# Five query tiles of 128, 128, 128, 96 and 96 rows, a new order of the first loads, and unread products at TensorE's start

## What is computed

```python
q_rot, k_rot = rotate(q), rotate(k)                  # (4, 8, 576, 64)
scores = (q_rot @ k_rot.T) / sqrt(64)
attn = exp(scores - max) / (sum(exp) + 1e-9)
x = (attn @ v) as (4, 576, 512)
u = x + (x.T @ U @ V).T                              # U (576, 32), V (32, 576)
out = u + maximum(u @ w_ch1, 0) @ w_ch2              # (512, 2048), (2048, 512)
```

## Time and profile before

| | |
|---|---|
| median of 3 executions | 755.5 us (755.38 to 759.19) |
| profiled execution | 755.52 us, span 753.7 us |
| TensorE busy | 712.1 us of the span |
| VectorE, ScalarE, GpSimd busy | 407.8, 438.8, 465.4 us |
| TensorE's first product | 11.00 us |
| scores of tile 5 (first of head 1) start | 24.59 us |
| first product with v starts | 30.34 us |
| scores of tile 10 (first of head 2) start | 34.13 us |
| MLP alone from | about 600 us |

### The profile page before, as it was taken

One profiled execution on the slowest core, in us unless ns is written; L12 is line 12 of the kernel. 1 busy time (PEld: TensorE's weight loads), 2 busy tenths in 40 slices (PEclk: granted clock), 3 DMA queues, 4 the chain that ended last, 5 costly groups with the idle time before them and its releaser, 6 DMA issues.

```text
span 753.7 us, 12305 instructions
## 1 busy us (share of the span) xinstructions
PE 712.1 (94%) x4292; PEld 640.9 (85%) x4292; DVE 407.8 (54%) x676; ACT 438.8 (58%) x948; POOL 465.4 (62%) x338
## 2 busy tenths in 40 slices
PE   3999987899999989999999999899999999999998
PEld 2888875799998879999999988788999889898986
DVE  5799997655556775344444566666555441112111
ACT  2788876676666666565565665667656343434341
POOL 4898865585668664664946867628433346565653
PEclk9999999999999999999999999999999999999999
DMA  7777675537474438348274373462623254434342
GB/s 208 196 210 201 190 208 153 179 95 207 129 228 134 140 126 246 131 144 241 85 220 165 103 209 131 139 191 79 160 70 107 69 196 137 165 128 168 127 167 72
DMA packets 73756, 117.82 MB, mean 156 GB/s; under 512 B 27040, under 2 KB 27168, under 8 KB 71904
## 3 DMA queue, kind: packets, MB, share of 16 engines
q1 hardware_dynamic: 73472, 116.68, 51.2%
q10 hardware_dynamic: 224, 0.36, 0.2%
HBM read 80.15 MB, written 9.44 MB: 119 GB/s over the span
## 4 chain that ended last, share of the span: by engine, by line
PE 75%; DVE 10%; ACT 7%; issue 5%; POOL 1%; DMA 1%; POOLq 0%; SPq 0%; ACTq 0%; DVEq 0%
PE ps L1131 25%; PE ps L1147 23%; PE ps L1045 8%; PE ps L1031 8%; PE ps L1065 6%; DVE negmax L865 3%; ACT prob L711 2%; PE ps L1058 1%; DVE ptl L874 1%; PE ps L1023 1%; ACT pth L722 1%; PE ps L1088 1%; DVE pth L878 1%; DMA raw<-in_qk 1%; PE ps L1113 1%
## 5 line engine op out<-in xcount | busy, mean ns | idle before, releaser
L650 POOL TENSOR_TENSOR w2l<-w2u,w2h 128x512 fp32r<-128x512 f32 x96 | 123.9, 1291 | 227.6 <-ACT w2h L775 227.6
L966 DVE SCALAR_TENSOR_TENSOR htl<-ps,hth 128x384 fp32r<-128x384 f32 x96 | 53.6, 558 | 183.9 <-ACT hth L782 183.6
L865 DVE TENSOR_REDUCE negmax<-ps 128x1 f32<-128x576 f32 (+1 forms) x160 | 120.2, 751 | 54.7 <-PE ps L1031 45.1
L711 ACT ACTIVATE prob<-ps,negmax 128x576 f32<-128x576 f32 (+1 forms) x160 | 117.9, 737 | 35.7 <-DVE negmax L865 34.4
L722 ACT ACTIVATE pth<-ps 128x512 fp32r<-128x512 f32 x156 | 87.5, 565 | 82.7 <-PE ps L1065 80.8
L1131 PE MATMUL ps<-ub,w1h 128*128 128x384 f32 x384 | 132.4, 345 | 2.2 <-DVE utl L957 2.2
L1131 PE MATMUL ps<-ub,w1l 128*128 128x384 f32 x384 | 129.5, 337 | 0.0
L1131 PE MATMUL ps<-utl,w1h 128*128 128x384 f32 x384 | 129.3, 337 | 0.0
L644 POOL TENSOR_TENSOR w1l<-w1u,w1h 128x512 fp32r<-128x512 f32 x96 | 123.7, 1289 | 6.7 <-ACT w1h L771 6.7
L782 ACT ACTIVATE hth<-ps 128x384 fp32r<-128x384 f32 x96 | 47.0, 490 | 136.9 <-PE ps L1131 136.7
L1031 PE MATMUL ps<-stack 128*128 128x288 f32 x620 | 113.3, 305 | 10.0 <-ACT prob L711 9.6
(11 more groups left out here) (81 smaller groups left out, 1127.0 us busy)
## 6 DMA issues: line engine op xcount, KB each, us to landing
w1u<-in_w SPq DMA_DIRECT2D x96, 256.0 KB, 2.6
w2u<-in_w SPq DMA_DIRECT2D x96, 256.0 KB, 2.6
stack<-raw SPq DMA_DIRECT2D x60, 288.0 KB, 4.5
raw<-in_qk SPq DMA_DIRECT2D x14, 1152.0 KB, 5.8
stack<-raw SPq DMA_DIRECT2D x60, 144.0 KB, 4.0
v2u<-in_v SPq DMA_DIRECT2D x16, 320.0 KB, 3.9
ubu<-scratch_u SPq DMA_DIRECT2D x18, 256.0 KB, 3.5
out<-ubu SPq DMA_DIRECT2D x18, 256.0 KB, 2.2
```

The costliest lines, as they stand in the source:

```text
L650: nc.gpsimd.tensor_tensor(w2l[:, at], w2u[:, at], w2h[:, at], ALU.subtract).then_inc(w2_lo, 1)
L711: nc.scalar.activation(tile_of(n, WT[t]).rearrange("p (c n) -> p c n", c=2), scores_of(n, WT[t]), ACT.Exp, bias=negmax[0:WT[t], t:t + 1], ...
L865: nc.vector.tensor_reduce(negmax[0:WT[t], t:t + 1], scores_of(n, WT[t]), AX.XY, ALU.max, negate=True).then_inc(maxed, 1)
```

## The change

Four edits:

1. The tiles become 128, 128, 128, 96 and 96 rows (WT), with QO for the first row of each. Slots, units and instructions keep their number and place. Unit 3 shrinks from 4 x 128 to 4 x 96 columns, LAST grows from 5 x 64 to 5 x 96, TAIL goes from 512 to 480 columns. The key tiles stay 128, 128, 128, 128 and 64.
2. SyncE's first loads wait for one another: k of pair 0; after the table, q of pair 0; after that, q of pair 1; then the k part of head 1's stack transfers; k of pair 1; the q part; and both loads of v.
3. GpSimd's wait for both low parts of pair 0 moves from between its multiply and its add of pair 1 to ahead of its first multiply.
4. TensorE begins with seven matmuls of 128 x 512 float32 (not rounded) on `hsum`, which VectorE fills with ones first. Their result, in PSUM bank 7, is never read.

```diff
-WT = [min(P, S - P * t) for t in range(NT)]
+KW = S - P * (NT - 1)
+FULL = 3
+WT = [P] * FULL + [(S - P * FULL) // (NT - FULL)] * (NT - FULL)
+QO = [sum(WT[:t]) for t in range(NT)]
+TURNED = QO[NT - 1]
...
             sp.dma_start(raw[:, 0, :, 1], qk[0][:, :, 1]).then_inc(first_loaded, 16)
+            sp.wait_ge(tables_loaded, 16)
             sp.dma_start(raw[:, 0, :, 0], qk[0][:, :, 0]).then_inc(raw_loaded[0], 16)
+            sp.wait_ge(raw_loaded[0], 16)
             sp.dma_start(raw[:, 1, :, 0], qk[1][:, :, 0]).then_inc(raw_loaded[1], 16)
-            sp.dma_start(raw[:, 1, :, 1], qk[1][:, :, 1]).then_inc(next_k, 16)
-            load_v(0)
             sp.wait_ge(lo_split[1], 1)
             stack_k(sp, 0, 1)
+            sp.dma_start(raw[:, 1, :, 1], qk[1][:, :, 1]).then_inc(next_k, 16)
             sp.wait_ge(lo_split[0], 1)
             stack_q(sp, 0, 1)
+            load_v(0)
             load_v(1)
...
-                if r == 1 and which == 0:
-                    for i in range(2):
-                        pool.wait_ge(lo_split[i], 1)
...
             pool.wait_ge(tables_twice, 1)
+            for which in range(2):
+                pool.wait_ge(lo_split[which], 1)
             prepare(1, ROPE_Q)
...
+            nc.vector.memset(hsum[:, :], 1.0).then_inc(filled, 1)
             dve.wait_ge(tables_loaded, 16)
...
+            pe.wait_ge(filled, 1)
+            for _ in range(WARM_UP):
+                nc.tensor.matmul(ps[:, 7 * BANK:8 * BANK], hsum[:, 0:P], hsum[:, :], start=True, stop=True)
             pe.wait_ge(ident_loaded, 16)
...
                     for t in range(NT - 1):
-                        mm = nc.tensor.transpose(bank[:, 0, P * t:P * t + P],
-                                                 prob[:, S * t + P * (NT - 1):S * t + S], ident[:, :])
+                        mm = nc.tensor.transpose(bank[:, 0, QO[t]:QO[t] + WT[t]],
+                                                 prob[0:WT[t], S * t + P * (NT - 1):S * t + S],
+                                                 ident[0:WT[t], 0:WT[t]])
```

More of the change, by code:

```diff
@@ L35 @@
 EARLY = 46
+WARM_UP = 7
 MERGED, LAGGED, MLP_FROM = 46, 51, 56
@@ L101 @@
 UT = 2 * S
-UT_NEEDED = [NT * ((TB * (p + 1) - 1) // S) + ((TB * (p + 1) - 1) % S) // P + 1 for p in range(NB)]
+UT_NEEDED = [NT * ((TB * (p + 1) - 1) // S) + sum(at <= (TB * (p + 1) - 1) % S for at in QO) for p in range(NB)]
 PARTS = [("up", 0, 0), ("up", 0, 1)]
@@ L396, in turned @@
         if j == TAIL:
-            return bank.rearrange("p (c n) -> p c n", c=1)[0:D], slice(NT - 1, NT), slice(0, BANK)
+            return bank[:, 0:TURNED].rearrange("p (c n) -> p c n", c=1)[0:KW], slice(NT - 1, NT), slice(0, TURNED)
         if j == LAST:
             return (bank[:, 0:NT * WT[-1]].rearrange("p (c n) -> p c n", c=NT), slice(0, NT),
-                    slice(P * (NT - 1), S))
-        return bank.rearrange("p (c n) -> p c n", c=NT - 1), slice(0, NT - 1), slice(P * j, P * j + P)
+                    slice(TURNED, S))
+        return (bank[:, 0:(NT - 1) * WT[j]].rearrange("p (c n) -> p c n", c=NT - 1), slice(0, NT - 1),
+                slice(QO[j], QO[j] + WT[j]))
     def pt_of(g):
@@ L413, in x_parts @@
     def x_parts(what, c):
-        rows, tiles = (P, slice(0, NT - 1)) if what == "pair" else (WT[-1], slice(NT - 1, NT))
+        rows, tiles = (P, slice(0, FULL)) if what == "pair" else (WT[-1], slice(FULL, NT))
         hi, lo = (x[:, :, :].rearrange("p x n -> p (x n)")[0:rows, PAIR * (c % 2):PAIR * (c % 2) + PAIR]
@@ L423, in ut_cols @@
     def ut_cols(b, t):
-        at = S * (b % 2) + P * t
+        at = S * (b % 2) + QO[t]
         return slice(at, at + WT[t])
@@ L1023, in scores @@
                             mm = nc.tensor.matmul(ps[0:WT[t], at + c * BANK:at + c * BANK + CH],
-                                                  first[0:D, 0, q, 0, P * t:P * t + WT[t]],
+                                                  first[0:D, 0, q, 0, QO[t]:QO[t] + WT[t]],
                                                   first[0:D, 0, k, 1, CH * c:CH * c + CH],
@@ L1031, in scores @@
                         mm = nc.tensor.matmul(ps[0:WT[t], at + c * BANK:at + c * BANK + CH],
-                                              stack[:, g % HEADS_STACKED, 0, P * t:P * t + WT[t]],
+                                              stack[:, g % HEADS_STACKED, 0, QO[t]:QO[t] + WT[t]],
                                               stack[:, g % HEADS_STACKED, part, CH * c:CH * c + CH],
@@ L1078, in mix @@
                         mm = nc.tensor.transpose(work(tenant, 0, rows, DM)[:, columns(i - tiles.start)],
-                                                 xt_of(b, t)[:, P * i:P * i + rows], ident[:, :])
+                                                 xt_of(b, t)[:, QO[i]:QO[i] + rows], ident[:, :])
                     mm.then_inc(nat_done, 1)
@@ L1085, in mix @@
                     for i in range(NT):
-                        _, tiles, hi, lo = x_parts("pair" if i < NT - 1 else "pair_end", t)
+                        _, tiles, hi, lo = x_parts("pair" if i < FULL else "pair_end", t)
                         for part in (hi, lo):
@@ L1094, in mix @@
                         mm = nc.tensor.transpose(work(tenant, 0, rows, DM)[:, P * c:P * c + P],
-                                                 xt_of(b, c)[:, P * t:P * t + rows], ident[:, :])
+                                                 xt_of(b, c)[:, QO[t]:QO[t] + rows], ident[:, :])
                     mm.then_inc(nat_done, 1)
@@ L1106, in mix @@
                     pe.wait_ge(h_ready, all_of(HIDDENS, b))
-                    mm = nc.tensor.matmul(work(tenant, 0, rows, DM), vs[:, P * t:P * t + rows], hs[:, :],
+                    mm = nc.tensor.matmul(work(tenant, 0, rows, DM), vs[:, QO[t]:QO[t] + rows], hs[:, :],
                                           start=True, stop=True)
@@ L1200 @@
     vp = np.ascontiguousarray(vp.reshape(B * PAIRS, NT, P, 2, D).transpose(0, 2, 1, 3, 4))
-    u4 = np.zeros((SP_, 4, R), moe_U.dtype)
-    u4[:S] = moe_U[:, None, :]
-    u4 = np.ascontiguousarray(u4.reshape(NT, P, P).transpose(1, 0, 2))
+    u4 = np.zeros((P, NT, 4, R), moe_U.dtype)
+    for t in range(NT):
+        u4[:WT[t], t] = moe_U[QO[t]:QO[t] + WT[t], None, :]
+    u4 = u4.reshape(P, NT, P)
     v4 = np.ascontiguousarray(np.concatenate([moe_V] * 4, axis=0))
```

12 lines of the change are left out of this document (6 added, 6 removed).

## The result

The changed kernel takes **747.9 us** (median of 4, 746.7 to 750.1) against 755.6 us before (median of 4, 755.4 to 759.2). The ratio is 0.989, with a 95% interval of 0.986 to 0.992: faster by 0.8 to 1.4%. The forecast was 751.4 us with a range of 749.0 to 755.2, so the gain of 7.6 us is nearly twice the forecast one and lies outside the range. The profiled execution took 748.9 us with a span of 747.0.

What follows compares the result with a forecast made beforehand. It took TensorE, busy 94% of the span, as the bound, with most of its unfilled time at the start. From 755.5 us, -4.4 at the first v product and +0.3 later gave 751.4 us, range 749.0 to 755.2.

Steps and rivals of the forecast that it cites:

- What bounds the kernel: Whole kernel: TensorE busy 94% of the span; most of what it does not fill lies at the start.
- the low parts (edit 3): Lead-in: with GpSimd held back, VectorE's two low parts of pair 0 take 0.75 us each, 2.35 us less.
- The loads (edit 2): Start: k lands near 5.3 us, q of pair 0 7.85, q of pair 1 11.6; about -0.2 us for VectorE.
- The unread products (edit 4): TensorE's start: seven products take 3.1 us if fast, 7.4 if slow, hidden; they gain 3 us or more, later hidden.
- rival B: Start: the unread products stay slow at 1.7 us each and no clock is won; 755.5 us, chance 0.08.
- What the products buy is the fast clock from the start: Lead-in: tiles take 1.74 us instead of 2.8, and tile 5 starts near 18 us instead of 24.59.
- Rival A: Lead-in: the fast clock does not hold, for tiles 1 to 7 or behind the v wait; 752.6 us, chance 0.17.
- GpSimd as the next gate: First v product: waits for GpSimd's low part of v, ready at 25.8 us; moves from 30.3 to 25.9, -4.4 us.
- The tiles (edit 1): All heads: equal sums of columns and equal instruction counts, so the new tile sizes gain nothing, 0 us.
- The prediction's own sign for this: Shifts at tile 30 and at the end differing by over 1 us would be the tiles' work.
- Rival D: Heads: even tiles regain part of VectorE's 0.32 us idle and shrink TensorE's waits; 749.5 us, chance 0.16.
- The sum: Whole kernel: -4.4 at the first v product plus 0.3 lost later gives -4.1 us, so 751.4 us.

Runs made afterwards that it cites:

- e6_oldpool: The changed kernel with GpSimd's wait for the low parts back between its first multiply and its add: 748.8 us (one execution).
- e4_warm9: The changed kernel with nine unread products at the start instead of seven: 749.5 us (one execution).
- e4_warm11: The changed kernel with eleven unread products at the start instead of seven: 751.5 us (one execution).
- e8_fill: The changed kernel with loads issued at once, nine unread products at the start and further 128 x 512 ones behind slots 0 to 4: 747.4 us.
- e11_halffill: The changed kernel with loads issued at once, nine unread products at the start and 128 x 256 ones behind slots 1 to 4: 746.8 us.
- e3_last96: The kernel before, with LAST's five transposes on 96 rows and columns (64 rows real, the rest zeros): 755.0 us, ratio 0.997.
- e10_last72: The kernel before, with LAST's five transposes on 72 rows and columns (64 rows real): 752.9 us (one execution).
- e1_tiles: The kernel before, with only the tiles changed to 128, 128, 128, 96 and 96 rows: 750.9 us, ratio 0.991.
- e5_nowarm: The changed kernel without the seven unread products and the fill of ones: 749.4 us, ratio 0.990.

## Why the prediction was wrong, and where it was right

**What bounds the kernel, and the low parts (edit 3): right.** Both low parts took 1.59 us, forecast 1.5, and with it 2.26 of the forecast 2.35 us were gained. e6_oldpool shows that edit 2 would have done it too, which the prediction had not seen: it priced the two edits apart.

**The loads (edit 2): the size was off.** k landed at 5.9, not 5.3: it got no faster for having less company. q of pair 0 was issued at 4.36 and took 4.0 us instead of 3.75, so it landed at 8.4 instead of 7.85, later than before (7.9). q of pair 1 landed at 12.6, not 11.6. So the term -0.2 was +0.4, and tile 0 gained 2.26 - 0.37 = 1.89 us.

**The unread products (edit 4): the failed step of the lead-in.** That they would be hidden was right: seven took 8.03 us, past the bounds of 3.1 and 7.4, but ended at 9.5, ahead of the scores. At the full clock one took 0.86 us (two records to a product, 0.43 us from start to start), at the slow rate 1.71 (0.853 from start to start up to 5.0 us), which is rival B's price. The 0.86 is twice the 0.44 that the rows on transposes gave. The Trainium skill (FP8 and Floating Point Precision, section TensorE Precision Notes) has four passes for true float32. An estimate from that is 4 x 512 columns at 2.4 GHz = 0.85 us, and the trace agrees with its 0.86. What failed is "What the products buy is the fast clock from the start". The clock fell in tile 0. Rival A had exactly this, at 0.17, and its first form: "tiles 1 to 7 go at 2.8 us again". Its argument against it, a wait of 1.7 us in the later stages that slowed nothing, was drawn from a stretch whose work around the wait is full of 128-row products; the lead-in's is not. e4_warm9 and e4_warm11 show that the pause alone is not the cause, e8_fill and e11_halffill that 128-row products between the tiles hold the clock.

**GpSimd as the next gate: right, but not reached.** In the changed kernel v was ready at 27.74 and TensorE came at 28.58, so nobody waited. In e11_halffill, with the clock held, the gate stood at 26.2 (forecast 25.9). The gain of -4.4 at this place was -4.1 there.

**The tiles (edit 1): the failed step of the whole.** "ScalarE's columns and those of the transposes have equal sums as well, with equal counts" is true, and I took a sum of columns for the cost of the transposes. The trace of before held the answer: four products ahead of LAST took 617 ns from start to start and 526 ahead of the others, and five transposes of 64 columns 454 where four of 128 take 356. I had added up columns, and not read the distance from start to start by shape. e3_last96 and e10_last72 show that it is not the columns, and the mixing's products on 64 rows and 128 columns that it is the rows: the term that was put at nothing measured -0.28 us a head (LAST and the scores ahead of it -0.18, unit 3 -0.10). The prediction's own sign for this came true: the shift is -2.25 at tile 30 and -6.65 at the end, "which would be the tiles' work". In the attention-only stage, where VectorE and GpSimd are as full as TensorE, the gain was only 0.07 us a head (e1_tiles, tiles 5 to 45) and not 0.27. There the forecast of nearly nothing held. Rival D ("1 to 2.5 us more") had the direction, but for a reason that isn't it (VectorE's idle time); the gain of the tiles was 6.5 us by the medians of e1_tiles, 3.9 at the end of its profile with two falls of the clock in it, and 6.5 in e8_fill without one (-8.2 at the end, -1.7 at tile 5).

**The sum.** -1.9 (lead-in) instead of -4.1; -0.8 (up to tile 50), +1.1 (the clock's fall at 131) and -5.1 (merged stages) instead of +0: -6.7, which is the difference of the two spans (753.7 and 747.0). The range stopped at 749.0, because the tiles were allowed to gain 2.6 us at most, VectorE's idle time, and the price of the transposes had no bound on the side of a gain.

**What stays open.** Why the clock falls near 110 to 135 and 590 us in some executions and not in others. In the changed kernel TensorE waits five times for ScalarE between 96 and 135 us,

```profile
PE ps L1045 <- ACT prob L720: 5.5, 5, 2.0
```

(us in total, times, longest), and nothing was tried against it. Which of the two, the short waits or the 64-row products, loses the clock in the lead-in: the fillers answer both at once. Why the weight load isn't taken ahead at the change to and from 64 rows. And why k took 5.1 us in either company.

## What to carry over

A column count prices a matmul group only when it overlaps with its neighbours. Read the time from the start of one group to the start of the next, by shape, before you say that equal sums cost the same, and look in the rows of the weight loads whether the next load begins under the running product. Where transposes of a tile of 64 rows stand between groups of 128, it is worth trying other tiles or a padded one. A warm-up buys the clock only if the work behind it keeps TensorE full: look at what the kernel does in the first tiles, and if it is thin, fill it, with less than the clock returns.

## What was not expected of the hardware

- The edges of a group on 64 rows cost 0.26 us more than those on 72: 617 ns ahead of it instead of 527, and 454 ns for five transposes of 64 columns where five of 72 take 283 (five of 96 on 96 rows: 361). The weight load at the edge begins 221 and 152 ns late instead of 4 and 2.
- The full clock was lost after a pause of 1.9 us and 0.4 us of 64-row scores; with nine unread products it was lost after 2.07 us of scores, a wait of 0.99 and 0.9 us of scores more, with eleven, and no pause, after 1.85, 0.98 and 0.5. In e6_oldpool it outlasted a pause of 1.13 us and 2.07 us of scores, and was lost 0.3 us into the wait of 0.99 behind them. With unread products of 128 rows and 256 columns between the tiles (0.6 us in every 2.0) it held.
- One fall of 3.4 us to half speed cost 1.1 to 1.6 us where the shifts of e1_tiles, e5_nowarm and the changed kernel show it, and nothing in e6_oldpool (at 116 us: tile 50 at -2.28, tile 60 at -2.49). The kernel before at clock 1.000 took 755.7 us and at 0.998 757.5 (medians), so the spread of 755 to 763 us in 20 executions goes with the number of falls.
- A load of 576 KB took 5.1 us with four loads issued right behind it, and 5.1 us with the first of them held back to 4.4 us and the others beyond its landing; with almost nothing beside it it took 4.0 to 4.2.
